# Six buffers for the bias copies of a three-stage attention kernel, and raw k and q of even heads in buffers of their own

## What is computed

```
B, H, S, D = 4, 8, 576, 64
scores = scale * np.matmul(q, k.transpose(0, 1, 3, 2))
psi_rel = np.log1p(np.abs(rel)); psi_i = np.log1p(np.maximum(pos[:, None], 1.0))
x = (psi_rel / psi_i)[..., None]
bias = np.maximum(x @ w1 + b1, 0.0) @ w2            # 576 x 576 for each of 8 heads
scores = scores + bias; attn = softmax(scores)
x = (attn @ v), heads side by side                  # 2304 tokens x 512
h = x @ w_in; x = (h - tanh(h)) @ w_out             # 512 -> 2048 -> 512
out = (silu(x @ w_gate) * (x @ w_val)) @ w_out2     # 512 -> 1536 -> 512
```

## Time and profile before

| What | Value |
|---|---|
| median of 3 runs | 1270.42 us (1266.47 to 1273.82) |
| the profiled execution's own time | 1269.69 us |
| its span, first to last instruction | 1267.7 us |
| bias stage, up to the first `score` of head 0 | 0 to 85.25 us |
| first unit, up to the first matmul of the feed-forward layer | 85.25 to 156.43 us |
| mean granted TensorE clock, share of full speed | 0.985 |

### The profile page before, as it was taken

How to read it: one execution, slowest core, us unless ns; L and a number is a source line. 1 busy time by engine, 2 the same in 40 slices (tenths; PEclk the granted TensorE clock), 3 DMA queues, 4 the chain that set the end, 5 groups by cost and what they waited for, 6 DMA issues and landing times.

```text
span 1267.7 us, 25030 instructions
## 1 busy us (share of the span) xinstructions
PE 1199.4 (95%) x8400; PEld 1130.5 (89%) x8400; DVE 637.4 (50%) x1575; ACT 595.1 (47%) x1301; POOL 573.8 (45%) x664
## 2 busy tenths in 40 slices
PE   5666799999999999999999999999999999999999
PEld 2335699999999999999999999999999999999998
DVE  7867778766666666666666654521211212112111
ACT  6766577655655655655556555521212222122212
POOL 1027689767677676666776644211111111111111
PEclk9989799999999999999999999999999999999999
DMA  4778444344444444444444424400000001000000
GB/s 155 203 218 268 139 154 124 113 141 122 140 120 120 139 120 120 139 120 121 135 123 123 132 87 169 143 26 1 25 26 25 25 10 40 0 26 1 26 1 25
DMA packets 69153, 125.01 MB, mean 99 GB/s; under 512 B 8544, under 2 KB 32096, under 8 KB 69088
## 3 DMA queue, kind: packets, MB, share of 16 engines
q1 hardware_dynamic: 69088, 124.16, 32.6%
HBM read 104.07 MB, written 20.05 MB: 98 GB/s over the span
## 4 chain that ended last, share of the span: by engine, by line
PE 83%; DVE 4%; ACT 3%; POOL 3%; issue 3%; DMA 2%; SPq 1%; POOLq 0%; DVEq 0%; ACTq 0%
PE ps_h L1101 14%; PE ps_y L1120 14%; PE ps_s L1192 12%; PE ps_y L1203 12%; PE ps_s L1054 6%; PE ps_h L1192 6%; PE ps_pt L1192 6%; PE ps_pt L1067 6%; PE ps_pt L1077 5%; DVE feat L825 1%; DMA bias_scratch<-x_stage 1%; POOL fr L529 1%; POOL prob L524 1%; PE ps_y L1077 1%; DVE prob L855 1%
## 5 line engine op out<-in xcount | busy, mean ns | idle before, releaser
L566 POOL TENSOR_TENSOR fr<-x_stage,fr 128x384 fp32r<-128x384 f32 x72 | 72.9, 1012 | 380.1 <-ACT fr L755 380.1
L524 POOL TENSOR_SCALAR prob<-prob,rowinv 96x576 f32<-96x576 f32 x192 | 149.6, 784 | 174.7 <-DVE rowinv L865 173.9
L1120 PE MATMUL ps_y<-fr,wbuf 128*128 128x288 f32 x1536 | 225.4, 295 | 1.1 <-POOL fr L529 0.4
L1101 PE MATMUL ps_h<-fr,wbuf 128*128 128x288 f32 x1440 | 220.1, 296 | 0.7 <-DVE fr L897 0.7
L1120 PEld LDWEIGHTS ps_y<-fr,wbuf 128*128 128x128 f32 x1536 | 210.3, 188 | 2.9 <-POOL fr L529 2.7
L1101 PEld LDWEIGHTS ps_h<-fr,wbuf 128*128 128x128 f32 x1440 | 201.2, 189 | 1.7 <-issue 1.1
L870 DVE TENSOR_TENSOR wbuf<-ps_pt,wbuf 128x480 fp32r<-128x480 f32 x176 | 115.6, 657 | 151.5 <-ACT wbuf L632 151.1
L632 ACT ACTIVATE wbuf<-ps_pt 128x480 fp32r<-128x480 f32 x176 | 100.5, 571 | 185.4 <-PE ps_pt L1067 185.1
L1203 PE MATMUL ps_y<-wbuf,fr 128*128 128x512 f32 x648 | 162.1, 395 | 0.0
L624 ACT ACTIVATE prob<-prob,negmax 96x576 f32<-96x576 f32 x192 | 147.8, 770 | 6.6 <-DVE negmax L855 6.5
L529 POOL TENSOR_TENSOR fr<-g_b,fr 128x288 fp32r<-128x288 f32 x128 | 112.1, 876 | 79.2 <-ACT fr L642 79.1
(11 more groups left out here) (109 smaller groups left out, 1832.8 us busy)
## 6 DMA issues: line engine op xcount, KB each, us to landing
biasb<-bias_scratch SPq DMA_DIRECT2D x192, 216.0 KB, 3.8
k_raw<-k_t SPq DMA_DIRECT2D x64, 288.0 KB, 2.8
v_raw<-v_p SPq DMA_DIRECT2D x64, 160.0 KB, 3.3
q_raw<-q_t SPq DMA_DIRECT2D x64, 144.0 KB, 2.6
w_raw<-w_chunks SPq DMA_DIRECT2D x16, 512.0 KB, 6.4
prob<-w_chunks SPq DMA_DIRECT2D x8, 768.0 KB, 4.3
bias_scratch<-x_stage SPq DMA_DIRECT2D x36, 144.0 KB, 2.4
bias_scratch<-y_stage SPq DMA_DIRECT2D x36, 144.0 KB, 2.6
```

Source lines behind the costliest of these rows:

```text
L524: eng.tensor_scalar(prob[0:QT, par, t, :], prob[0:QT, par, t, :], rowinv[0:QT, par, t:t + 1], 1.0, ALU.mult, ALU.mult).then_inc(p_norm, 1)
L1101: mm = eng.matmul(hidden_bank(u, c)[:, 0:T1], w[:, cols], x[:, d, :], start=d == 0 and i == 0, stop=d == KC - 1 and i == 2)
L1120: mm = eng.matmul(ps_y[:, d, 0:T1], w[:, cols], g[c % 2], start=c == 0 and i == 0, stop=c == C1 - 1 and i == 2)
```

## The change

Three things are changed. First, `bias_ev` gets six buffers (`EV`), in the room of the raw weight chunks 8 to 11 (`w1_raw[4]` and `w1_raw[5]`), and ScalarE waits for the stores of six pairs earlier in place of two; six semaphores in place of two say that stores have landed. Second, k and q of the even heads of the first unit (0, 2, 4, 6, 8) get raw buffers and semaphores of their own, in the room of chunks 12 and 13 (`w1_raw[6]`), so that the load of head n waits for the splits of head n-2; k and q of head 1 are loaded at the start. Third, the bias rows of head 1 are loaded behind the last store in place of behind the store of round 27, and both loads wait for the stores that they read.

```diff
-        bias_ev = [t[:, :, :].rearrange("p (q a) n -> p q (a n)", q=2) for t in (x_stage, y_stage)]
+        raw_even = w1_raw[6][:, :, :, :, :].rearrange("p c i s n -> p (c i s n)")[:, 2 * S + 2 * T1:]
+        k_raw_even, q_raw_even = raw_even[:, 0:S], raw_even[:, S:S + T1]
+        bias_ev = [w1_raw[4 + i][:, :, :, :, :].rearrange("p c i s n -> p (c i s n)")[:, j * 2 * S:(j + 1) * 2 * S]
+                   .rearrange("p (q n) -> p q n", q=2) for i in range(2) for j in range(3)]
...
+        def raw_free(n):
+            return n - 1 if isinstance(n, int) and n <= H + 1 else n
...
             def store_bias(rnd):
-                i = rnd // 2 % 2
+                i = rnd // 2 % EV
...
             def load_q(n):
-                wait(eng, v_q, n)
+                wait(eng, v_q, raw_free(n))
...
             def load_k(n):
-                wait(eng, p_klo, n)
+                wait(eng, p_klo, raw_free(n))
...
-            load_k(0)
-            load_q(0)
+            for n in range(2):
+                load_k(n)
+                load_q(n)
             load_v(0)
...
-                if rnd == 11:
-                    load_k(1)
-                    load_q(1)
             for rnd in range(W1_LOADS, NQUAD, 2):
                 store_bias(rnd)
                 if rnd == W1_LOADS:
+                    for i in range(EV):
+                        eng.wait_ge(d_bias_out[i], 64 * (1 + (EV + i < NQUAD // 4)))
                     load_bias(0, 0)
-                    load_bias(1, 1)
                     load_k(2)
                     load_q(2)
-            for i in range(2):
-                eng.wait_ge(d_bias_out[i], 64 * (NQUAD // 4))
+            load_bias(1, 1)
+            for i in range(EV):
+                eng.wait_ge(d_bias_out[i], 64 * (NQUAD // 2 // EV))
...
             def evacuate(rnd):
-                if rnd >= 4 and par == 0:
-                    eng.wait_ge(d_bias_out[rnd // 2 % 2], 64 * (rnd // 4))
-                eng.activation(pairs(bias_ev[rnd // 2 % 2][:, par, :]), bias_ps[par][:, :, 0:T1], ACT.Identity,
+                if rnd >= 2 * EV and par == 0:
+                    eng.wait_ge(d_bias_out[rnd // 2 % EV], 64 * (rnd // 2 // EV))
+                eng.activation(pairs(bias_ev[rnd // 2 % EV][:, par, :]), bias_ps[par][:, :, 0:T1], ACT.Identity,
```

More of the change, by code:

```diff
@@ L50 @@
 W2_STAGES = 3
+EV = 6
 BIG = 3.0e38
@@ L157, in attention_layers_kernel @@
         d_q, d_k, d_v = sem("d_q"), sem("d_k"), sem("d_v")
+        d_q_even, d_k_even = sem("d_q_even"), sem("d_k_even")
         d_bias = [sem("d_bias0"), sem("d_bias1")]
-        d_bias_out, d_y_out, d_y_in, d_out = [sem(f"d_bias_out{i}") for i in range(2)], sem("d_y_out"), sem("d_y_in"), sem("d_out")
+        d_bias_out, d_y_out, d_y_in, d_out = [sem(f"d_bias_out{i}") for i in range(EV)], sem("d_y_out"), sem("d_y_in"), sem("d_out")
         pool_tab, dve_tab, dve_rest, dve_b, act_tab = (sem(x) for x in ("pool_tab", "dve_tab", "dve_rest", "dve_b", "act_tab"))
@@ L272, in operands, with own_raw, raw_count @@
             return (q_one if isinstance(n, int) and n == 1 else qq), k_hi, k_lo
+        def own_raw(n):
+            return isinstance(n, int) and n <= H and n % 2 == 0
+        def raw_count(n):
+            if isinstance(n, int) and n <= H:
+                return 16 * (n // 2 + 1)
+            return n * 16 - 16 * (H // 2)
+        def raw_free(n):
+            return n - 1 if isinstance(n, int) and n <= H + 1 else n
         def score_bank(par, t, moe):
@@ L358, in load_q @@
             def load_q(n):
-                wait(eng, v_q, n)
+                wait(eng, v_q, raw_free(n))
                 bh, half = n % (B * H), n // (B * H)
-                eng.dma_start(q_raw[:, :], q_t[bass.ds(bh * 2 + half, 1), :, :].rearrange("o p n -> (o p) n"))\
-                   .then_inc(d_q, 16)
+                eng.dma_start(q_raw_even if own_raw(n) else q_raw[:, :],
+                              q_t[bass.ds(bh * 2 + half, 1), :, :].rearrange("o p n -> (o p) n"))\
+                   .then_inc(d_q_even if own_raw(n) else d_q, 16)
             def load_k(n):
-                wait(eng, p_klo, n)
-                eng.dma_start(k_raw[:, :], k_t[bass.ds(n % (B * H), 1), :, :].rearrange("o p n -> (o p) n"))\
-                   .then_inc(d_k, 16)
+                wait(eng, p_klo, raw_free(n))
+                eng.dma_start(k_raw_even if own_raw(n) else k_raw[:, :],
+                              k_t[bass.ds(n % (B * H), 1), :, :].rearrange("o p n -> (o p) n"))\
+                   .then_inc(d_k_even if own_raw(n) else d_k, 16)
             def load_v(n):
@@ L501, in split_k @@
             def split_k(n, par, moe):
-                eng.wait_ge(d_k, n * 16 + 16)
+                eng.wait_ge(d_k_even if own_raw(n) else d_k, raw_count(n))
                 _, hi, lo = operands(n, par, moe)
@@ L506, in split_k @@
                 hold(eng)
-                eng.tensor_scalar(hi, k_raw[:, :], 1.0, 1.0, ALU.mult, ALU.mult).then_inc(p_khi, 1)
+                raw = k_raw_even if own_raw(n) else k_raw[:, :]
+                eng.tensor_scalar(hi, raw, 1.0, 1.0, ALU.mult, ALU.mult).then_inc(p_khi, 1)
                 eng.wait_ge(p_khi, n + 1)
-                eng.tensor_tensor(lo, k_raw[:, :], hi.bitcast(F32), ALU.subtract).then_inc(p_klo, 1)
+                eng.tensor_tensor(lo, raw, hi.bitcast(F32), ALU.subtract).then_inc(p_klo, 1)
             def split_v(n, first=False):
@@ L576, in q_high @@
             def q_high(n, par, moe):
-                eng.wait_ge(d_q, n * 16 + 16)
+                eng.wait_ge(d_q_even if own_raw(n) else d_q, raw_count(n))
                 wait(eng, e_score, preparing(n, moe))
-                eng.activation(operands(n, par, moe)[0], q_raw[:, :], ACT.Copy, scale=float(D) ** -0.5).then_inc(a_q, 1)
+                eng.activation(operands(n, par, moe)[0], q_raw_even if own_raw(n) else q_raw[:, :], ACT.Copy, scale=float(D) ** -0.5).then_inc(a_q, 1)
             def evacuate(rnd):
@@ L830, in q_low @@
                 eng.wait_ge(a_q, n + 1)
-                eng.scalar_tensor_tensor(q[64:P, :], q_raw[64:P, :], float(D) ** -0.5, q[64:P, :].bitcast(F32),
+                raw = q_raw_even if own_raw(n) else q_raw[:, :]
+                eng.scalar_tensor_tensor(q[64:P, :], raw[64:P, :], float(D) ** -0.5, q[64:P, :].bitcast(F32),
                                          ALU.mult, ALU.subtract).then_inc(v_q, 1)
```

## The result

| | before | after |
|---|---|---|
| median, run side by side | 1269.85 us (6 runs) | 1258.92 us (6 runs; 1256.5 to 1261.7) |
| ratio | | 0.9916, 95% interval 0.9893 to 0.9939 |
| profiled execution; span | 1269.69; 1267.7 us | 1256.5; 1254.4 us |

The account below looks back on a forecast made before the run. VectorE paces the bias stage, losing time behind ScalarE's waits for stores. 15.53 us less 0.75 for the split and 1.9 for head 1's wait gives 12.9, plus 1.97: 14.9 off 1269.69, so 1255 us, range 1249 to 1264.

Parts of the forecast that it names:

- Steps 1 and 2: Bias stage: VectorE's features without gaps, then a tail of 2.05 us; last copy at 69.60 us, 15.53 us earlier.
- Step 3: Start of bias stage: GpSimd's early split of head 1's k delays VectorE's tables by 0.75 us (0 to 1.5).
- Step 4: First `score` of head 1 waits 1.9 us (0.4 to 3.7) for bias rows now loaded behind the last store.
- rival B: Bias stage: DMA queue falls behind at 240 GB/s, head 1's wait becomes 8.0 us, 1261 us; chance 0.15.
- Step 5: First unit: ScalarE no longer waits for q, slots of heads 2 and 5 shorten, 1.97 us gained.
- What was counted as nothing: First unit: output matmuls meeting the lower clock may change, 1.2 us each, up to three heads either way; counted 0.
- rival E: First unit: the half-clock output matmuls vanish as well, 1249 us; chance 0.07.

Follow-up runs that it names:

- e1: Kernel before with the six bias buffers alone and the waits the loads then need: 1257.96 us, ratio 0.9909.
- e2: Changed kernel with the old two bias buffers, the other two parts kept: 1268.16 us, ratio 0.9989.
- e4: Changed kernel with GpSimd's split of k of head 1 held until VectorE's features are done: 1256.95 us.
- f5: Changed kernel with head 1's rows early, k and q of head 3 earlier, the early split held, only weight chunks 0 and 1 in the bias stage: 1252.64 us.
- e5: Changed kernel with weight chunks 8 to 11 loaded one per head behind heads 4 to 7, not two behind heads 4 and 5: 1258.79 us.
- e3: Changed kernel with head 1's bias rows loaded behind the store of round 27 again: 1258.64 us.
- e7: Changed kernel with three bias buffers instead of six: 1259.12 us.
- e6: Changed kernel with the edits of e3, e4 and e5 together: 1257.66 us.
- f3: Changed kernel with head 1's rows early, k and q of head 3 behind those of head 2, the wait for all stores moved to head 4: 1254.42 us.
- f7: f6 with four filler matmuls in place of eight ahead of each of seven outputs, and twelve ahead of the eighth: 1249.91 us.
- f6: Changed kernel with loads reordered, early split held, weight chunks 4 to 11 left to the first unit, plus eight filler matmuls ahead of seven outputs: 1253.09 us.

## Why the prediction was right, and where it was off

**The forecast by its own steps.** 1255 us with a range of 1249 to 1264 was forecast, 1258.92 came, for the reason given: the six buffers.

**Steps 1 and 2, right.** ScalarE waits for no store, VectorE is all but without gaps from 20 us on (0.2 us in all), TensorE stays at a granted clock of 1.00. The features end 1.1 us later than forecast (69.41 for 68.3), the tail takes 2.11 us for 2.05. e1 and e2 show that the whole gain hangs on this. That ScalarE needs less for a round than VectorE holds only just (53.19 and 55.38 us busy).

**Step 3, too small.** 0.75 us was taken, with bounds of 0 and 1.5. The features of round 1 start 1.41 us later: 0.27 us from 0.46 to 0.73, 1.08 us from 0.66 to 1.74, and 0.06 of small ones. Behind the very first round, TensorE's next ones take 2.16, 2.14 and 1.95 us in place of 1.21, three of them where before it was two, and so the two gaps at 18.22 and 19.97 us, 0.36 and 0.20 us, are new. The granted clock column shows 1.00 there, so what slows them is not shown; nor is it the split, for e1, without an early split, has the same gaps (0.36 and 0.23 us). e4, with both gone, has h0 2.16 us earlier. By the rule of the Trainium skill, SBUF — State Buffer, section Who interferes with whom, that a VectorE instruction with two SBUF inputs and one of GpSimd lock each other out for a whole instruction, the prediction had up to 2.2 us; the trace, with 1.08 us beside GpSimd's 1.44, agrees in kind.

**Step 4, too small.** 1.9 us was taken with an upper bound of 3.7; it was 3.62, and h1 at 79.84 us is just under the 80 that would have meant rival B. The term that failed is the issue of the last store: forecast by 72.1 us, it was 74.2. Of this 1.2 us are the later copy, by which `score` is later too; the other 1.0 us is SP. Head 0's loads and k and q of head 2 hold SP until 65.2 us, so it comes to the next stores 2.5 us behind their copy, at 62.70 us, and at 0.56 us each in place of 0.43 it does not catch up; step 4 had taken these stores as not held. The landing of the third load, 4.26 us, was near the median used; it was issued 0.2 us later behind the last store than forecast. So B held in part: the schedule of step 4 needed 272 GB/s and the queue moved 250. That the full queue is what slows the issues is not shown: f5, with fewer bytes ahead, took 10.41 us for the same 16 stores.

**Step 5, wrong.** The failed step: "ScalarE no longer waits for q, since its load is issued a head earlier." It is issued earlier only if SP gets there. SP stands at the load of v, which waits for GpSimd (32.3 us in all, the longest 5.2), and k and q stand behind it, behind the bias rows and one or two chunks of 512 KB. Their landing rose from medians of 3.6 and 3.7 us to 6.1 to 7.1. In the slot of head 2 the first two `score` still lie 2.60 us apart (2.63), in that of head 5 2.30 (3.82), and in that of head 4 3.69, where it was 2.61: 0.03 + 1.52 - 1.08 = 0.47 us in place of 1.97. e5 shows the chunks' part: one per head, and the waits for q of heads 5 and 6 go.

**What was counted as nothing.** Half-clock outputs went from three and a part to one and a part, 2 x 1.18 = 2.4 us, rival E in part. (By the prediction's own price, up to three outputs at 1.2 us, E comes to 1251.4 us; its 1249 is not worked out.) So the whole is 13.61 - 3.59 + 0.47 + 2.4 = 12.9 us of the 13.05 at the first feed-forward matmul. The sum of the steps was 4.4 us too good (1.2, 1.7 and 1.5), and 2.4 us of clock hid part of that. e1 and e3 to e7 have three to five outputs of 2.1 us or more with the same code there, so the changed kernel's profile was a good draw; its median lies 2.4 us above it.

**What was late next** the prediction didn't see: the place of k and q of head 3 on SP, behind the wait for all stores, three loads of rows and a chunk. Step 4 had the rows behind that wait "some 4 us later, well ahead of `score` of head 2"; that held for the rows in the changed kernel (with head 1 earlier, in e1, e3 and e6, `score` of head 2 waited for them 1.3 to 2.4 us), but k and q of head 3, behind them in order, were not counted. e6 and f3 show it: in e6 three waits were shortened and 1.3 us won in the medians; in f3, without e4 and e5, k and q of head 3 were taken out of that place, and 4.5 us won. The intervals of the two overlap; q of head 3 at 80.95 us in place of 86.32 doesn't leave it open. How much of it is the wait alone is not shown; SP stands in it for 2.4 us in e6, where q is waited for 7.03.

Not tried: the wait for all stores moved by itself, why the first rounds are slow, and loads from a second engine's queue.

## What to carry to other kernels

When a buffer is made deeper, the next limit is the in-order queue that serves it: follow every load that stands behind the new burst, and ask what each wait in that queue holds that doesn't need it. Small edits that each remove a wait and win nothing point to one common wait behind them all; find the instruction whose start does not move. Where an engine with an activity-dependent clock idles for a known time ahead of a piece on the path, a filling that is shorter than the gap can hold the higher level; in f7 1.0 us in gaps of 1.3 us did, seen in the profile.

## What the runs showed of the hardware

SP's issue of a 144 KB store took 0.42 us in the median in both kernels, single ones up to 1.72 us before and 1.35 us after; in the last 16 of the changed kernel it was 0.56 us on average, in those of f5 0.65. Behind SP's burst the landing of k and q went from 3.6 to 3.7 us to 6.1 to 7.1 us at nearly the same rate (250 GB/s before from 85 to 112 us, 264 after from 72 to 102 us), which fits a longer queue, not a slower one. A 128 x 96 product in float32 counted as two instructions and took 0.24 us (1.92 / 8).

With 1.3 us of idle time ahead of it, an output of the first unit was at a granted clock of 1.00 or 0.50 in the same run; with that time filled, all 15 filled outputs of f6 and f7 took 1.56 to 1.59 us. The Trainium skill, TensorE: Matmul & The Clock Gate, section Part 1: The HAM clock gate, says that the low level is the default and that activity releases it; f6 and f7 agree.
